# One step of ScalarE's hand-written loop is moved behind its neighbour

## The reference

```python
# x (4, 3008, 256), w_r and w_i (256, 256), b_r and b_i (256)
X = np.fft.rfft(x, axis=1)                      # along the 3008 positions
Yr = Xr @ w_r - Xi @ w_i + b_r
Yi = Xr @ w_i + Xi @ w_r + b_i
Y  = soft-threshold of Yr and Yi by 0.01
y  = np.fft.irfft(Y, n=3008, axis=1)            # (4, 3008, 256)

h = y.reshape(12032, 256) @ w_in                # w_in (256, 2048)
P = a[0] + a[1] * h + a[2] * h**2 + a[3] * h**3
Q = 1.0 + abs(b[0]) * abs(h) + abs(b[1]) * h**2
out = (P / (Q + 1e-06)) @ w_out                 # w_out (2048, 256)
```

## Time and profile before

| | |
|---|---|
| median of three runs | 1424.05 us (1423.68 to 1426.2) |
| profiled execution, its own time | 1424.05 us |
| its span | 1422.2 us |
| around the span | 1.85 us |
| TensorE matmul busy | 1381.5 us, 97% |
| TensorE weight load busy | 972.5 us, 68% |
| VectorE busy | 1331.7 us, 94% |
| ScalarE busy | 1243.0 us, 87% |
| GpSimd busy | 632.6 us, 44% |
| mean granted TensorE clock | 0.995 of full |

### The profile page before, as it was taken

How to read it: one execution, slowest core, us unless ns; L and a number is a source line. 1 busy time by engine, 2 the same in 40 slices (tenths; PEclk the granted TensorE clock), 3 DMA queues, 4 the chain that set the end, 5 groups by cost and what they waited for, 6 DMA issues and landing times.

```text
span 1422.2 us, 21592 instructions
## 1 busy us (share of the span) xinstructions
PE 1381.5 (97%) x7498; PEld 972.5 (68%) x7498; DVE 1331.7 (94%) x1639; ACT 1243.0 (87%) x1654; POOL 632.6 (44%) x417
## 2 busy tenths in 40 slices
PE   7998999999999999999999999999999999999987
PEld 3875677777767677677777776776766666666666
DVE  5687999999999999999999999999999999999998
ACT  4577999998888998988989988988889999999986
POOL 0001544444444444444445445444445555555554
PEclk9999999999999999999999999999999999999999
DMA  8976756656556656555555555565455545555443
GB/s 280 289 234 143 169 130 146 152 133 137 119 136 138 143 138 133 127 117 122 108 130 113 129 115 126 108 137 115 95 115 112 109 89 116 109 118 109 85 95 71
DMA packets 97913, 188.07 MB, mean 132 GB/s; under 512 B 11216, under 2 KB 57744, under 8 KB 97808
## 3 DMA queue, kind: packets, MB, share of 16 engines
q0 software_dynamic: 29952, 98.58, 37.5%
q1 hardware_dynamic: 67856, 88.12, 20.8%
HBM read 50.60 MB, written 37.49 MB: 62 GB/s over the span
## 4 chain that ended last, share of the span: by engine, by line
PE 66%; DVE 19%; ACT 6%; issue 6%; DMA 2%; POOL 1%; SPq 0%; ACTq 0%; POOLq 0%
PE h_ps L564 23%; PE o_ps L594 8%; PE o_ps L579 8%; PE o_ps L581 8%; DVE den L1092 4%; DVE num L1098 4%; DVE num L1112 4%; DVE g_hi L1087 4%; PE d L541 3%; PE d L505 3%; PE d L481 2%; PE d L475 2%; ACT sq L791 1%; POOL g_lo L1175 1%; ACT num L794 1%
## 5 line engine op out<-in xcount | busy, mean ns | idle before, releaser
L1175 POOL TENSOR_TENSOR g_lo<-num,sq 128x940 fp32r<-128x940 f32 (+1 forms) x205 | 471.0, 2297 | 91.4 <-DVE num L1098 90.8
L1167 POOL DMA_DIRECT2D den<-sq x208 | 182.5, 877 | 685.7 <-ACT sq L791 382.1
L579 PE MATMUL o_ps<-g_hi,wout_hi 128*128 128x470 f32 (+1 forms) x832 | 342.4, 412 | 0.9 <-DVE g_hi L1087 0.9
L581 PE MATMUL o_ps<-g_hi,wout_lo 128*128 128x470 f32 (+1 forms) x832 | 310.7, 374 | 0.0
L564 PE MATMUL h_ps<-yt_hi,win_hi 128*128 128x470 f16 (+1 forms) x832 | 301.4, 362 | 4.7 <-DVE num L1115 4.7
L564 PE MATMUL h_ps<-yt_lo,win_hi 128*128 128x470 f16 (+1 forms) x832 | 299.4, 360 | 0.0
L564 PE MATMUL h_ps<-yt_hi,win_lo 128*128 128x470 f16 (+1 forms) x832 | 299.4, 360 | 0.0
L1112 DVE TENSOR_TENSOR num<-h_ps,num 128x940 f32<-128x940 f32 (+1 forms) x208 | 232.1, 1116 | 27.8 <-ACT num L794 26.9
L1115 DVE SCALAR_TENSOR_TENSOR num<-num,coef,h_ps 128x940 f32<-128x940 f32 (+1 forms) x208 | 245.1, 1179 | 7.4
L1092 DVE SCALAR_TENSOR_TENSOR den<-den,g_hi 128x940 f32<-128x940 f32 (+1 forms) x208 | 244.2, 1174 | 0.2
L1087 DVE SCALAR_TENSOR_TENSOR g_hi<-num,a_sb,sq 128x940 fp32r<-128x940 f32 (+1 forms) x208 | 244.3, 1174 | 0.0
(11 more groups left out here) (167 smaller groups left out, 1571.3 us busy)
## 6 DMA issues: line engine op xcount, KB each, us to landing
den<-sq POOLq DMA_DIRECT2D x200, 470.0 KB, 4.4
z_in<-spec SPq DMA_DIRECT2D x96, 128.0 KB, 2.9
spec<-s_out SPq DMA_DIRECT2D x96, 128.0 KB, 2.8
xw<-in_x SPq DMA_DIRECT2D x31, 384.0 KB, 4.8
out_t<-o_sb SPq DMA_DIRECT2D x25, 470.0 KB, 4.6
spec<-s1w SPq DMA_DIRECT2D x56, 192.0 KB, 3.0
zp_in<-spec SPq DMA_DIRECT2D x22, 480.0 KB, 5.0
inv_in<-in_inv SPq DMA_DIRECT2D x96, 64.0 KB, 2.3
```

The source lines that it names most:

```text
L579: pe.matmul(o_ps[:, h, 0:w], wout_hi[:, f, h * P:(h + 1) * P], g_hi[q % 3][:, j, 0:w], start=f == 0, stop=False)
L581: mm = pe.matmul(o_ps[:, h, 0:w], wout_lo[:, f, h * P:(h + 1) * P], g_hi[q % 3][:, j, 0:w], start=False, stop=False)
L1175: pool.tensor_tensor(g_lo[r % 2][:, :, 0:cols(r)], ring(num, r), ring(sq, r), ALU.mult).then_inc(n_g, 1)
```

## The change

In ScalarE's loop, `evacuate_s4` moves from between rs and rec to behind rec. Nothing else in the program changes.

```diff
                 if q < NS:
                     act.wait_ge(s_q[q % 4], 16 * (q // 4 + 1))
                     act.activation(ring(sq, q), ring(den, q), ACT.Abs_reciprocal_sqrt, bias=qone[:, 0:1]).then_inc(n_rs, 1)
-                if q - 3 in S2_AT:
-                    evacuate_s4(S2_AT[q - 3], d0[:, :])
                 if q < NS:
                     act.wait_ge(n_rs, q + 1)
                     act.activation(ring(sq, q), ring(sq, q), ACT.Square).then_inc(n_rec, 1)
+                if q - 3 in S2_AT:
+                    evacuate_s4(S2_AT[q - 3], d0[:, :])
                 if q and q in S1_AT:
                     sum_abs(S1_AT[q])
```

## The result

The changed kernel takes 1435.2 us (median of four runs, 1433.38 to 1437.82) against 1424.86 us for the one before on the same chip: ratio 1.0068, 95% interval 1.0056 to 1.0081, that is 8.0 to 11.5 us slower. The record has twenty executions of the changed kernel from this measurement, 1432.68 to 1437.82 us; their median is 1434.4 us, and the ratio goes with that one, since 1435.2 alone would make 1.0073. The profiled execution took 1435.4 us, its span 1433.5 against 1422.2.

The account below looks back on a forecast made before the run. TensorE was taken as the bound up to about 1050 us, VectorE behind it. Stalls of 4.5, 2.9 and 1.0 us, less 0.32 absorbed, gave 1424.05 + 8.1 = 1432.2 us; 8-in-10 range 1427 to 1434.5.

Parts of the forecast that it names:

- the stall: Slots 3 of tiles: later s_out delays s5, 0.645 us mean in seven with s1, 0.31 to 0.48 in seven without.
- slot 75: Its 0.32 us stall was to go into TensorE's 0.76 us gap at 644.02, costing nothing.
- TensorE sets the pace: Up to about 1050 us TensorE has no slack, so each us it is made to stand lengthens the kernel.
- The rival built on the Trainium skill's rule: VectorE is the bound; earlier rec brings `num` forward and cuts its waits: 10 us faster, 1414; chance 6%.
- What ScalarE gains is worth 0: Where s_out waited for s4 (50 slots), rec fills the wait, up to about 0.9 us sooner; costed at 0.
- Slot 131: No s3 covers s_out, so s5 already waits; it would start at 991.25 instead of 990.26: 1.0 us.
- The fall of the clock: At slot 131 the longer idle gap drops TensorE to 1.2 GHz: 1.8 us more, 1434.0; chance 10%.
- The sum: Stalls of 4.5, 2.9 and 1.0 us make 8.4, net +8.1 with slot 75's 0.32 us absorbed.
- The alternative sum with 0.093 us of overlap for both pairs: Using the skill's overlap for rs and rec and for rec and s_out, the stalls sum to about 6.5 us.

Follow-up runs that it names:

- e1: Kernel before with rec ahead of s_out only in slots 3 of the tiles, old order elsewhere: ratio 1.0075 to the kernel before, 10.7 us slower.
- e2: Kernel before with rec ahead of s_out everywhere but in slots 3 of the tiles: ratio 0.9997 to the kernel before, -0.4 us.
- e6: Kernel before, old order, with a useless 940-column ScalarE instruction ahead of s_out in slots 3: ratio 1.0047, 6.7 us slower.
- e9: Kernel before with the new order only in slots 75, 83, 91, 99, 107, 123 and 139: ratio 1.0024, 3.4 us slower.
- e10: The changed kernel run again unaltered, to look at the clock behind slot 131: 1433.32 us, one run.
- e3: The changed kernel with the old order kept in slot 131: ratio 1.0059 to the kernel before, 8.4 us slower.
- e5: Kernel before, old order, with a useless 256-column ScalarE instruction ahead of s_out in slots 3: ratio 1.0001.
- e7: Kernel before with s4 between the halves of f1 in slots 113 and 131, s_out ahead of rs in 131: ratio 0.9986, 2.0 us faster.

## Why the prediction was wrong, point by point

The mechanism, the places and the sign were right: 1432.2 was forecast, and 1435.2 lies 0.7 us above the range. One term was mis-sized, the stall, 1.3 us low in all; slot 75 was wrongly taken as absorbed, 0.3 us low; a gain put at nothing made 0.5 us the other way; and the rest, 1.9 us, is not a step of the sum.

- **TensorE sets the pace.** Right, by e1, e2, e6 and e9. The rival built on the Trainium skill's rule (Perfetto Trace Analysis, "Identifying the Most-Contended Engine") was wrong here: the engine with 94% occupancy was not the one whose time counts, and the engine with 68% by weight loads was.
- **What ScalarE gains is worth 0.** Right to 0.5 us. The eight pairs of steps that cancel show it at work: `num` is done 0.54 to 0.59 us earlier and one or two slots later nothing is left. The one gain that stays is at slots 113 to 114. Before, GpSimd's long `g_lo` of slot 112 lay beside L1092, TensorE waited 0.23 us for it and L1092 took 1.82 us:

```profile
870.42 1.82 DVE L1092 SCALAR_TENSOR_TENSOR den<-den,g_hi 128x940 f32<-128x940 f32 x1
...
871.29 1.13 PE L594 MATMUL o_ps<-g_lo,wout_hi 128*128 128x470 f32 x4 [0.23 <-POOL g_lo L1175]
```

  In e10, with the new order, L1092 takes 1.30 us and L594 follows without a gap:

```profile
877.57 1.30 DVE L1092 SCALAR_TENSOR_TENSOR den<-den,g_hi 128x940 f32<-128x940 f32 x1
...
878.03 1.02 PE L594 MATMUL o_ps<-g_lo,wout_hi 128*128 128x470 f32 x4
```

  The whole step lies at this L594, 0.38 us in its start and 0.11 us behind it. The first profile, e2 and e3, which all have the new order outside slots 3, have it too, and e1, which has not, does not. That the earlier work of ScalarE moved the overlap is read from the order of times, and no run isolates it.
- **The stall at each s5.** Its start was forecast well: 0.62 us late in slot 11 by the sum, 0.62 to 0.63 by the trace (s5 starts at 200.57 instead of 199.93, and TensorE's matmuls ahead of it stand 0.01 to 0.02 us later). Two of the working's values show side by side in the rows above, rec's lag behind rs (0.03 us) and the overlap behind rec (0.10). **The step that failed** is the one that priced a stall at its length, from the moment when TensorE would have come to s5's first matmul. TensorE comes to the first weight load before that, and a load that waits is no longer hidden: 0.10 us in 13 of the 14 new stalls, 1.3 us in all. It was there to be read: the waiting s5 of the earlier trace rows is 1.35 us long, those of slots 11, 67 and 139 in the earlier trace rows 1.25. Slot 75 is the exception, with 1.33 us before and 1.35 behind the change. Its load stood only 0.03 us ahead of the matmul at 633.90:

```profile
632.65 0.48 ACT L762 ACTIVATE s_out<-d,x_inv 128x256 f32<-128x256 f32 x1
```

```profile
633.87 1.20 PEld L541 LDWEIGHTS d<-c_sb,zp_in 96*128 96x128 f32 x10
```

  Counted up to the first weight load, the rows of the kernel before give the whole cost. Slot 11: 1.02 - (199.82 - 199.48 - 0.05) = 0.73, measured 0.72 to 0.74. Slot 75: 1.02 - (633.87 - 633.13 - 0.05) = 0.33, measured 0.30 to 0.33. The same working for all 15 slots makes 9.7 us, and with the -0.5 us of slots 113 to 114 that is the 9.2 us of the loop.
- **Slot 75 was to be absorbed** by the gap at 644.02. It was not: +0.30 us. I took VectorE's unbroken row of work for a chain that starts before the stall. It had no slack towards ScalarE. Before and after the change:

```profile
637.08 1.18 DVE L1098 SCALAR_TENSOR_TENSOR num<-num,a_sb,den 128x940 f32<-128x940 f32 x1
638.28 0.42 DVE L974 SCALAR_TENSOR_TENSOR ythr<-d,neg 128x256 f32<-128x256 f32 x1
```

```profile
642.27 1.18 DVE L1098 SCALAR_TENSOR_TENSOR num<-num,a_sb,den 128x940 f32<-128x940 f32 x1
643.79 0.42 DVE L974 SCALAR_TENSOR_TENSOR ythr<-d,neg 128x256 f32<-128x256 f32 x1 [0.34 <-ACT neg L751]
```

  TensorE's stall makes s5, `yt_hi` and then `neg` late, and L974 waits 0.34 us for it. An engine without idle time can still be just in time behind another.
- **Slot 131.** The stall was right (1.0 forecast, 1.0 measured). The fall of the clock, given 10%, came in one of six traces, at 1.5 us where 1.8 was forecast.
- **The sum**: 8.1 + 0.3 + 1.3 - 0.5 = 9.2 us, against 9.1 to 9.3 in the loops of the three later traces of the changed kernel. So 1.1 us of the miss are the sum's. About 1 us is the base's: the 1424.05 us of the forecast were the median of three runs, and the later medians of the kernel before are 1424.86 to 1425.19. Outside the loop the profiled execution before was a short one as well: in the twelve other traces the part before slot 0 took 0.8 us less to 2.5 us more and the part behind slot 207 up to 0.9 us more. Base and loop together make 1434.1 to 1434.4, and the twenty executions have a median of 1434.4. The last 0.8 us, up to the 1435.2 of four of them, is chance. How often the clock fell at slot 131 among the twenty is open, since only one was traced.
- **The range** was drawn for errors of 0.14 us in each stall and for the clock, but with no room for the base or for how executions differ outside the loop. The median of the twenty, 1434.4, lies just inside its upper end of 1434.5 and that of the four outside. That is luck in either direction; the price of the stall was wrong in both cases.
- **Smaller readings.** In slots 1, 5 and 7 ScalarE waits for s4 up to 1.56 us and not up to 1.1, which changes nothing. Slot 139 was worked out with 1.47 where the others have 1.45; its s5 starts 0.44 us late against the 0.48 forecast. The alternative sum with 0.093 us of overlap for both pairs comes to 6.8 (15 x 0.123 less, 15 x 0.017 more than 8.4) and not 6.5.

## What to carry to other kernels

Filling one engine's wait is worth nothing where that wait is for the engine that sets the pace; look instead at what the moved instruction releases. Here a result handed to TensorE must be ready when TensorE comes to it. The room can be read slot by slot as the time from the end of the copy to the start of the first weight load, less the 0.05 us from release to start (0.29 us in slot 11). Moves within it are free, and what goes beyond it costs in full.

When a stall is put on TensorE, measure it from the weight load, which no longer hides behind the matmul before, and not from the matmul. Before counting on a gap further on to absorb it, check that the engine that makes the gap does not itself hang on what is delayed: busy without a pause is not the same as ahead.

## What the runs showed of the hardware

Between 140 and 1400 us, and at the entry into the loop near 130 us, the granted clock falls six times in the thirteen traces. Each time it is just behind one of three gaps of TensorE, and most times the same gap has no fall behind it:

| gap of TensorE | traces with it | clock fell behind it | cost of the fall |
|---|---|---|---|
| 1.95 us near 130 us, waiting for VectorE | 13 | 3 (e3, e5, e7) | none: shift within 0.03 us |
| 1.57 to 1.58 us at slot 131, waiting for s_out | 6 | 1 (first profile) | 1.5 us |
| 1.80 to 1.82 us at 1062 to 1072 us, waiting for GpSimd | 13 | 2 (before, e6) | none: see below |

What the slow matmuls cost depends on what follows. At slot 131 TensorE is dense behind the gap. At the other two places it soon waits again: near 135 us about 1.2 us for VectorE, and near 1068 to 1079 us about 1.25 us for GpSimd. In the traces in which the clock fell this second wait is gone, and the time with it. So the kernel before has the fall at 1062 us and the changed one has not (granted clock 1.00):

```profile
1070.00:1080.00 10.00, 6.93 (x33) 4.19 (x32) 9.86 (x14) 7.34 (x8) 5.23 (x3) 1.00 0.39 74
```

and yet the shift between them stays within 0.1 us from slot 142 to slot 207. What decides between fall and no fall behind the same gap is not shown by these runs.

A VectorE instruction of one form and size (L1092, 128x940) took 1.13, 1.30 or 1.82 us in the rows above, the long ones where GpSimd's `g_lo` ran beside it. Over the whole trace before, 106 of them with under 0.1 us of such overlap took 1.13 to 1.14 us, 33 with 0.3 to 0.4 us took 1.30 to 1.37 us, and five with over 0.8 us took 1.48 to 2.05 us. GpSimd's spans are rough in a profile, and no run here was made to separate the two.
